# An attention and expert kernel on one core: masks written per head, all scores in one visit, softmax steps moved behind other groups

## What is computed

```python
# attention: a pooled one (means over 4 positions, 144 x 144) and a banded one
out_up    = np.repeat(sm_attn(q_d, k_d, v_d), 4, axis=2)
mask      = np.abs(pos[:, None] - pos[None, :]) < 4
scores    = np.where(mask, scale * q @ k.T, -1e9)
out_local = softmax(scores) @ v
x = (out_up + out_local)            # -> (1152, 512)
# layer 1: 512 -> 2048 -> 512
h = x @ w_in ; x = np.where(h > 0, h, np.exp(np.minimum(h, 0)) - 1) @ w_out
# layer 2: 4 experts, each 512 -> 1024 -> 512, weighted by p
out += p[:, e:e+1] * (np.maximum(x @ w1[e], 0) @ w2[e])
```

## The kernel before, in words

| step | j = 0 | j = 1 | j = 2 |
|---|---|---|---|
| scores on PE, behind group | 3 | 3 | 5 |
| maxima on DVE, in group | 3 | 4 | 5 |
| exponentials on ACT, in group | 3 | 4 | 6 |
| reciprocals on DVE, in group | 4 | 5 | 7 |
| turns on PE, behind group | 7 | 9 | 11 |

## Time and profile before

### The profile page before, as it was taken

How to read it: one execution, slowest core, us unless ns; L and a number is a source line. 1 busy time by engine, 2 the same in 40 slices (tenths; PEclk the granted TensorE clock), 3 DMA queues, 4 the chain that set the end, 5 groups by cost and what they waited for, 6 DMA issues and landing times.

```text
span 653.5 us, 12960 instructions
## 1 busy us (share of the span) xinstructions
PE 643.8 (99%) x4698; PEld 593.1 (91%) x4698; DVE 346.3 (53%) x764; ACT 286.8 (44%) x778; POOL 324.1 (50%) x282
## 2 busy tenths in 40 slices
PE   8999999999999999999999999999999999999998
PEld 5788999999999999998998898899899899889986
DVE  5866454545466876774544554453454355365342
ACT  4878383838385686564233133142062152142210
POOL 4674434344388799998326237037056065160200
PEclk9999999999999999999999999999999999999999
DMA  9954333423112132302103003002012021020012
GB/s 179 240 116 138 102 104 89 116 53 115 64 66 68 65 127 64 111 19 68 64 0 129 1 1 128 0 34 94 0 64 64 0 64 64 1 64 1 2 49 96
DMA packets 51491, 46.13 MB, mean 71 GB/s; under 512 B 31616, under 2 KB 33920, under 8 KB 51456
## 3 DMA queue, kind: packets, MB, share of 16 engines
q1 hardware_dynamic: 51456, 45.67, 24.2%
HBM read 43.30 MB, written 2.36 MB: 70 GB/s over the span
## 4 chain that ended last, share of the span: by engine, by line
PE 90%; ACT 5%; DVE 4%; issue 1%; ACTq 0%; DVEq 0%
PE psum L500 15%; PE psum L502 15%; PE psum L501 15%; PE psum L573 11%; PE psum L575 11%; PE psum L577 11%; PE psum L643 2%; PE psum L642 2%; PE psum L641 2%; ACT attn L853 1%; PE psum L492 1%; DVE neg_max L1189 1%; ACT attn_p L853 1%; PE psum L423 1%; PE psum L486 1%
## 5 line engine op out<-in xcount | busy, mean ns | idle before, releaser
L1603 POOL TENSOR_TENSOR wb_lo<-wb_raw,wb_hi 128x512 fp32r<-128x512 f32 x64 | 81.7, 1295 | 185.1 <-ACT wb_hi L887 185.1
L1413 DVE SCALAR_TENSOR_TENSOR o_acc<-psum,gate_now,o_acc 128x512 f32<-128x512 f32 x72 | 54.0, 751 | 127.1 <-PE psum L502 127.0
L502 PE MATMUL psum<-wb_hi,h_lo 128*128 128x512 f32 x288 | 112.3, 390 | 0.0
L501 PE MATMUL psum<-wb_lo,h_hi 128*128 128x512 f32 x288 | 112.3, 390 | 0.0
L500 PE MATMUL psum<-wb_hi,h_hi 128*128 128x512 f32 x288 | 112.1, 389 | 0.0
L997 ACT ACTIVATE h_hi<-psum 128x320 fp32r<-128x320 f32 (+1 forms) x128 | 52.4, 411 | 87.4 <-DVE psum L1385 40.3
L1603 POOL TENSOR_TENSOR wa_lo<-wa_raw,wa_hi 128x512 fp32r<-128x512 f32 x60 | 77.5, 1315 | 16.9 <-ACT wa_hi L928 16.9
L1003 ACT COPY sums<-psum 128x256 f32<-128x256 f32 (+1 forms) x32 | 12.8, 400 | 155.1 <-PE psum L577 155.1
L577 PE MATMUL psum<-x_hi,wa_lo 128*128 128x256 f32 (+2 forms) x228 | 67.4, 296 | 0.0
L575 PE MATMUL psum<-x_lo,wa_hi 128*128 128x256 f32 (+2 forms) x228 | 67.3, 295 | 0.0
L573 PE MATMUL psum<-x_hi,wa_hi 128*128 128x256 f32 (+2 forms) x228 | 67.3, 295 | 0.0
(11 more groups left out here) (194 smaller groups left out, 1682.9 us busy)
## 6 DMA issues: line engine op xcount, KB each, us to landing
wa_raw<-in_moe_w_in SPq DMA_DIRECT2D x8, 1024.0 KB, 5.5
wb_raw<-in_moe_w_out SPq DMA_DIRECT2D x8, 1024.0 KB, 5.0
wa_raw<-in_moe_w SPq DMA_DIRECT2D x8, 1024.0 KB, 5.0
wb_raw<-in_moe_w SPq DMA_DIRECT2D x8, 1024.0 KB, 5.1
out<-o_acc SPq DMA_DIRECT2D x9, 256.0 KB, 2.0
q_in<-in_q SPq DMA_DIRECT2D x10, 144.0 KB, 4.7
k_in<-in_k SPq DMA_DIRECT2D x10, 144.0 KB, 4.3
v_in<-in_v SPq DMA_DIRECT2D x5, 288.0 KB
```

Source lines behind the costliest of these rows:

```text
L501: nc.tensor.matmul(bank_cols, w_hi(n), x_lo_(n), start=False, stop=False)
L502: last = nc.tensor.matmul(bank_cols, w_lo(n), x_hi_(n), start=False, stop=(n == chunks - 1))
L1413: nc.vector.scalar_tensor_tensor(o_acc[:, m, :], psum[:, DOWN2_BANKS[(MT * half + m) % 2], :], gate_now[:, m:m + 1], o_acc[:, m, :], ALU.m ...
L1603: nc.gpsimd.tensor_tensor(lo[:, c, :], raw[:, c, :], hi[:, c, :].bitcast(F32), ALU.subtract).then_inc(lo_ready, 1)
```

## The change

The mask of a band call is written head by head, from a `band` and an `ident2` that both have 128 rows: head h multiplies rows and columns 64h to 64h + 63, as the products behind it do. `band` is now one strip of 144 columns from which each chunk takes 72, at an offset; chunks with the same offset are written together (`BAND_RUNS`), so a call has two runs for two heads, four bf16 matmuls in place of one. This holds for both modes. In MIXED mode all three score calls come behind group 3. ACT's exponentials move from groups 3, 4, 6 to groups 4, 6, 8, DVE's reciprocals from 4, 5, 7 to 5, 7, 9, DVE's copy of the turned pooled weights from 8 to 9, and PE's turns from behind groups 7, 9, 11 to behind 8, 10, 11. The maxima stay in groups 3, 4 and 5. GpSimd's constants at the start need two selections for the band in place of six.

```diff
+BAND_RUNS = (None, ((0, 1), (1, 4)), ((4, LAST), (LAST, NQT)))
+BAND_PAD = QT * LAST - WIN_START[LAST]
-        band = sb1("band", [QT, NQT, WIN], BF16)
+        band = sb1("band", [128, BAND_PAD + QT + WIN], BF16)
-        ident2 = sb1("ident2", [QT, 2 * QT], BF16)
+        ident2 = sb1("ident2", [128, 128], BF16)
+        def band_of(h, c0, c1):
+            at = BAND_PAD + QT * h - (QT * c0 - WIN_START[c0])
+            run = band[HD * h:HD * (h + 1), at:at + WIN]
+            return run if c1 == c0 + 1 else run.unsqueeze(1).to_broadcast([HD, c1 - c0, WIN])
...
-                    nc.tensor.matmul(psum[:, bank, 0:(c1 - c0) * WIN], ident2[:], band[:, c0:c1, :], start=True, stop=False)
+                    for n, (e0, e1) in enumerate(BAND_RUNS[j]):
+                        for h in range(2):
+                            rows = slice(HD * h, HD * (h + 1))
+                            nc.tensor.matmul(psum[QT * h:QT * (h + 1), bank, WIN * (e0 - c0):WIN * (e1 - c0)],
+                                             ident2[rows, rows], band_of(h, e0, e1), start=(n == 0), stop=False,
+                                             skip_group_check=True)
...
                         score(u, 0, MIXED)
                         score(u, 1, MIXED)
-                    elif g == 5:
                         score(u, 2, MIXED)
-                    elif g in (7, 9, 11):
-                        turn_attn(u, (g - 7) // 2, MIXED)
+                    elif g in (8, 10, 11):
+                        turn_attn(u, (8, 10, 11).index(g), MIXED)
...
-                    3: [(exponentiate, u, 0, MIXED)],
-                    4: [(exponentiate, u, 1, MIXED)],
-                    6: [(exponentiate, u, 2, MIXED)],
+                    4: [(exponentiate, u, 0, MIXED)],
+                    6: [(exponentiate, u, 1, MIXED)],
+                    8: [(exponentiate, u, 2, MIXED)],
...
-                    4: [(row_max, u, 1, MIXED), (reciprocals, u, 0)],
-                    5: [(row_max, u, 2, MIXED), (reciprocals, u, 1)],
-                    7: [(reciprocals, u, 2)],
-                    8: [(copy_attnT_p, u, MIXED)],
+                    4: [(row_max, u, 1, MIXED)],
+                    5: [(row_max, u, 2, MIXED), (reciprocals, u, 0)],
+                    7: [(reciprocals, u, 1)],
+                    9: [(reciprocals, u, 2), (copy_attnT_p, u, MIXED)],
...
-                for c0, n in ((0, 1), (1, NQT - 2), (NQT - 1, 1)):
-                    part = band[:, c0, :] if n == 1 else band[:, c0:c0 + n, :]
...
+                nc.gpsimd.affine_select(out=band[:], in_=band[:], compare_op=ALU.is_ge, fill=MASKED,
+                                        base=sign * BAND_PAD + FACTOR - 1, pattern=[[-sign, BAND_PAD + QT + WIN]],
+                                        channel_multiplier=sign).then_inc(const_step, 1)
```

More of the change, by code:

```diff
@@ L433, in score @@
                                                     qT[slot(u)][rows, QT * c:QT * (c + 1)], kT[slot(u)][rows, s:s + WIN],
-                                                    start=False, stop=(c == c1 - 1))
+                                                    start=False, stop=(c == c1 - 1), skip_group_check=True)
                 last.then_inc(scored, 1)
@@ L1660, in _ @@
             nc.gpsimd.affine_select(out=ident2[:], in_=ident2[:], compare_op=ALU.not_equal, fill=1.0, base=0,
-                                    pattern=[[0, 2], [-1, QT]], channel_multiplier=1).then_inc(const_step, 1)
+                                    pattern=[[-1, 128]], channel_multiplier=1).then_inc(const_step, 1)
             nc.gpsimd.memset(band[:], 0.0).then_inc(const_step, 1)
             for step, sign in enumerate((1, -1)):
-                pool.wait_ge(const_step, 4 + 3 * step)
-                for c0, n in ((0, 1), (1, NQT - 2), (NQT - 1, 1)):
-                    part = band[:, c0, :] if n == 1 else band[:, c0:c0 + n, :]
[L1668 to L1672, removed]
+                pool.wait_ge(const_step, 4 + step)
+                nc.gpsimd.affine_select(out=band[:], in_=band[:], compare_op=ALU.is_ge, fill=MASKED,
+                                        base=sign * BAND_PAD + FACTOR - 1, pattern=[[-sign, BAND_PAD + QT + WIN]],
+                                        channel_multiplier=sign).then_inc(const_step, 1)
+            pool.wait_ge(const_step, 6)
             pool.sem_inc(band_ready, 1)
```

## The result

| | before | after |
|---|---|---|
| median | 654.93 us (4 runs, 654.62 to 655.47) | 650.58 us (4 runs, 650.11 to 650.80) |
| ratio | | 0.9932, 95% interval 0.9914 to 0.9949 |
| profiled execution, own time | 655.29 us | 650.72 us |
| its span | 653.5 us | 648.9 us |

A forecast was written before the change was run, and what follows sets the result against it. From 44 us on, PE's own stream and its standstills were taken as the bound. 2.7 us plus 1.4 (2.6 less 1.2) makes 4.1 off the median of 654.71: 650.6 us, range 649.0 to 652.8.

The forecast's parts named there:

- Part 1, the visits: PE's score visits in mixed blocks: masks by head and one joint visit save 0.67 us a pair, 2.7 us together.
- Part 2, the wait before group 7: PE's wait for group 3's low part in the mixed blocks goes with the new order: 2.6 us, net 1.4.
- The new wait before group 8: PE before group 8 in mixed blocks: 0.18 us late, 0.29 with the longer first step, 1.2 us lost over four blocks.
- Moved steps: Later exponentials, reciprocals and turns in the mixed blocks cost nothing, with 1.4 us of cover for the turn of j = 2.
- Stage one: First 44 us: masks don't stand in the chain, so 0, with ends of 0.5 us gained and 0.5 lost.
- Rival C: ACT and DVE's chain before groups 7 and 8 0.5 us longer: 3.6 us of waits, 654.2 us; chance 0.10.
- D: Score visits: each of a pair's eight mask matmuls stands alone, 8.3 us lost in four blocks, 658.8 us; chance 0.05.
- Rival A: Before group 8: no new wait, so the 1.2 us stay gained, 649.4 us; chance 0.15.
- B: Score visits: masks not side by side (1.1 us), or bf16-fp32 mixing costs 1.6 us; 651.7 to 652.2 us; chance 0.15.

The follow-up runs named there:

- Experiment 6: Changed kernel with DVE's reciprocals of j = 0 moved from group 5 to group 6: 649.62 us, ratio to before 0.9915.
- experiments 1 and 2: Kernel before with masks by head alone (1: 655.04 us, ratio 0.9996), or with these and one score visit, old order (2: 655.29 us, ratio 0.9999).
- experiment 7: Experiment 6 with the turns of j = 0 and j = 1 both behind group 10 and DVE's copy in group 10: 650.27 us, ratio to before 0.9926.
- experiment 4: Changed kernel with the old masks, one bf16 matmul of 64 rows by 128 columns a call: 652.86 us, ratio to before 0.9959.

## Why the prediction was right

- **Part 1, the visits: 2.7 us.** Right: one visit of 2.32 us where 1.76 + 1.23 stood, 0.67 a pair. Its terms are right too: with the masks alone the two visits are 0.25 and 0.09 us shorter, where 0.24 was forecast for the first, and joining them brings the other 0.33. The masks ran side by side, at 0.13 and 0.16 us. The rule of the Trainium skill that was weighed against this ("TensorEngine Tiling (Array Packing)", Restrictions and Gotchas: different row tiles cannot access the same PSUM bank simultaneously) isn't borne out by these runs, for bf16 no more than for fp32: both heads' masks write one bank.
- **Part 2, the wait before group 7: 2.6 us.** Right: the order alone takes 2.62 us off. Group 7's low part starts at 121.42 in the kernel after, G + 4.18 where 4.24 was forecast (G is the start of group 4, 117.24).
- **The new wait before group 8: 1.2 us.** Right in place and in what ends it, a size was off. It was put at 0.18 us late and 0.11 of slow step in each block. It measured 0.07 and 0.10 in the loop blocks, and 58.41 against 58.25 us, 0.16 and 0.08, in the first: together 0.75. The loop blocks' chain came out 0.09 us shorter than its sum of eleven distances (group 8 at G + 6.56, not 6.65). That is the 0.4 us by which the mixed stretch shrank more, 4.53 against 4.1. Experiment 6, which removes this wait and gains 0.79 us, confirms size and cause.
- **Moved steps: nothing.** Right. POOL's multiplication for j = 2 runs from 129.23 to 130.02 us and the turn of its first chunks is due at 131.3: 1.3 us of cover, 1.4 forecast.
- **Stage one: nothing.** It can't be told. It ended 0.09 us earlier in the profiled execution, but the executions of this study spread over 0.8 us there.
- **The two parts as separate terms.** The sum is right and would mislead whoever took one term alone. The 2.7 us of part 1 exist only behind part 2: without the new order they are worth nothing (experiments 1 and 2), with it the masks by head are worth 1.4 in two visits and 1.9 in one. The prediction held this implicitly, by working out the chain of ACT and DVE from group 4's start, but said nowhere that part 1 alone would be worth nothing.

**What is luck.** 650.58 us measured against 650.6 is closer than the forecast was. The gain in the mixed stretch was 4.5 us, not 4.1; the median of the kernel before was 654.93 us in the comparison, 0.22 above the 654.71 that the sum starts from. The first puts the sum 0.4 us too high, the second 0.2 us too low, and the scatter of the medians did the rest.

**Slips that moved nothing.** Rival C's price counts its delay twice. By the prediction's own chain, 0.5 us more would start group 8 at G + 7.15 instead of 6.65, and what PE waits before group 7 is part of these 0.5 us: 2.0 us over four blocks, 652.6 us, and not 3.6 and 654.2. C as priced would still have been faster than before. In D, 8 x 0.29 is 2.32, not 2.35; by that its 658.8 us stands. The waits in PEld's list were to become about 1 us: they are 0.5 in the first profiled execution of the kernel after and 1.0 in the other.

Rival A's time, no wait before group 8, is 1.2 us less by the forecast's own numbers and 0.8 by what was measured. B, C and D didn't come about: no mask was slower than its columns, group 7 doesn't wait, and none of the masks stands alone.

## What to carry to other kernels

Where an engine waits at one point in each turn of a loop, work taken from it ahead of that point may be worth nothing until the wait is gone, as in experiments 1 and 2; follow the other engines' chain from its own last wait on that engine, and see whether the saving comes before or after it. Small steps of one engine that stand ahead of the step which frees a buffer are worth moving: two small DVE operations, one group later, were worth 0.8 us. Before a visit is moved or joined with another, look for a wait, or a close arrival, that it hides.

## What the runs showed of the hardware

- A layer step of PE whose bank comes free just too late, or just in time, costs more than the lateness: it is 0.21 to 0.24 us long instead of 0.13 when it is 0.06 to 0.16 us late (group 8 in the kernel after), and 0.21 when it isn't late at all (group 9 in experiment 7). In the trace this is a longer first record (0.37 to 0.40 us instead of 0.29) with no idle time beside it.
- bf16 matmuls among fp32 ones in the same 64*64 shape change places without a gap: 0.13 and 0.16 us for 288 and 360 columns a head, within 0.01 us of the column price of the earlier trace rows. A change between 64*64 and 64*128 costs about 0.1 us each way and 0.05 in the step behind: the visit with four such changes is 2.79 us long in experiment 4, and 2.32 without them.
